# A one-core kernel of attention and two feed-forward layers: local attention regrouped from 64-key windows to blocks of 24 queries by 32 keys

## The chip, the core and the metric

The kernel runs on one core of one Trainium2 chip. The metric is the device time of one execution in microseconds (us). A core has TensorE (PE in the profile, its weight loads PEld), VectorE (DVE), ScalarE (ACT), GpSimd (POOL) and SyncE (SP, which here only issues DMAs). The engines run side by side and are kept in order by semaphores that the program counts by hand.

## What is computed

Attention of 4 batches x 8 heads, 576 positions, 64 wide, in two parts that are added; then two feed-forward layers over the 2304 tokens. Everything is fp32. Condensed:

```python
def _attn_ref(q, k, v):
    factor = 4; Sd = S // factor; scale = 1.0 / np.sqrt(D)
    q_d = q.reshape(B, H, Sd, factor, D).mean(axis=3)      # k_d, v_d alike
    out_d = sm_attn(q_d, k_d, v_d)                         # 144 x 144 softmax attention
    out_up = np.repeat(out_d, factor, axis=2)
    mask = np.abs(pos[:, None] - pos[None, :]) < factor    # local: 7 keys a query
    scores = np.where(mask, scale * q @ k.T, -1e9)
    out_local = softmax(scores) @ v
    return out_up + out_local
def _moe_ref(x, w_in, w_out):                              # 512 -> 2048 -> 512
    h = x @ w_in; return (h * tanh(softplus(h))) @ w_out   # Mish
def _moe2_ref(x, w_in, w_out, g_ln):                       # 512 -> 1024 -> 512
    h = x @ w_in; return (layernorm(h * softmax(h)) * g_ln) @ w_out
```

## The kernel before

**Stages.** Attention runs first, over 16 units (`UNITS`); a unit is two heads (2 x 64 = 128 partitions) of one batch. The first feed-forward layer follows in 6 tiles of 384 tokens by 16 blocks of hidden columns, then the second in 9 pairs of token tiles. Both layers are matmuls in fp32r, three per product (high and low parts), and their lines are not touched, save for the order of one Mish.

**Local attention of a unit.** A query sees the keys up to 3 positions away. The 576 queries are cut into 10 blocks of 58 (`QB`); each looks at a window of 64 keys (`KW`). `score_local` adds the mask into PSUM with 4 bf16 matmuls (L601), then computes 10 x 2 heads = 20 matmuls of 64 rows by 64 queries by 64 keys (L607) on the four 64x64 quarters of the array. In the profile an fp32 matmul that isn't a transpose has two records, so L607 shows 40 a unit. The scores of a unit are 128 x 640. VectorE takes the row maxima (L1099), subtracts them (L1102) and sums the exponentials (L1109); ScalarE exponentiates (L868); GpSimd normalises (L506). TensorE turns the result with 5 transposes (L631), ScalarE copies it (L863), and `value_local` multiplies by the values in `vw` with 20 matmuls of 64 keys by 64 columns by 58 queries (L657, 40 records). VectorE evicts in two copies of 128x290 (L1127).

**Pooled attention of a unit.** Queries, keys and values are summed in fours. GpSimd pools the queries (L485, L488), of every second unit also the keys; VectorE pools the other keys (L1064, 9 in all). GpSimd pools V from `v8`, 72 partitions of 8 rows each (L498, L499), so that each partition yields two pooled rows, g = 0 and 1. `score_pooled` is 6 matmuls (L588, 12 records), `turn_pooled` 6 transposes (L623), `value_pooled` 4 matmuls with 72 rows (L642, 8 records), two for each head.

**Order on TensorE.** It is written out by hand. In round u of 18 (`UNITS + LATE`) TensorE runs `turn_pooled` and `turn_local` of unit u-2, `score_local` and `score_pooled` of unit u, then `value_pooled` and `value_local` of unit u-2. In rounds 16 and 17, where there is nothing left to score, hidden blocks 0, 1 and 2 of the first layer (L671, 12 matmuls each) are put in.

**Order on the sync queue.** In round s: q and k of unit s (L405, L406), the values of unit s-3 into `vw` in 4 DMAs (L388) after a wait for `l_valued`, then `v8` of unit s-2 (L412) after a wait for `pool_v`.

**Mish.** ScalarE's `mish(0, 0)` stands in round 16; `mish(0, 1)` comes in the loop behind it, after weight block 4 and, because of `act.wait_ge(x_ok, UNITS)`, after the last eviction. There are two banks for hidden blocks, so `hidden(0, 3)` waits for `mish(0, 1)`.

Of the kernel before, what the change touches and what calls it, by code (L numbers as in the profile page):

```python
# [5 lines left out]
ALU = mybir.AluOpType  # L6
ACT = mybir.ActivationFunctionType
AX = mybir.AxisListType
# [17 lines left out]


KW = 64
QB = KW - 2 * (POOLF - 1)
NP = 5  # L30
NB = 2 * NP
PSTEP = 2 * QB - 1
LW = NP * KW

# [5 lines left out]
PQ = POOLED // 2  # L40
# [43 lines left out]
def first_query(i, jp):  # L84
    return PSTEP * i + QB * jp


def half_rows(h, jp):

    return slice((h ^ jp) * HD, (h ^ jp) * HD + HD)  # L90


def window(i, jp):

    return min(max(first_query(i, jp) - (POOLF - 1), 0), SEQ - KW)


def first_row(i, jp):

    return min(first_query(i, jp), SEQ - KW)  # L100

# [6 lines left out]
def program(nc, qT_d, kT_d, v_d, w1_d, w2_d, gln_d, out_d):  # L108
    with ExitStack() as ctx:
# [37 lines left out]
        v8 = sb("v8", [PQ, 2, 8 * P])  # L147
        qd = sb("qd", [P, 2, QPAD])
        kd = sb("kd", [P, 2, POOLED])
        vd = sb("vd", [PQ, 2, 2, P])  # L150
        half_qk = sb("half_qk", [P, 2, 2 * POOLED])
        half_v = sb("half_v", [PQ, 4 * P])
        band = sb("band", [P, 2, 2, KW], BF16)
# [4 lines left out]
        prob = sb("prob", [P, 2, NP, 2, KW])  # L158
        probT = sb("probT", [P, NP * P])
        pprob = sb("pprob", [P, 2, NPB, POOLED])  # L160
        vw = sb("vw", [P, 2, NP, P])
# [14 lines left out]
        pprobT = sb("pprobT", [PQ, 2, NPB, 2, PB])  # L176
        maskb = sb("maskb", [P, NB, KW], BF16)
        identb = sb("identb", [P, P], BF16)
        eps = sb("eps", [P, NB + NPB])
        mx = sb("mx", [P, 2, NP])  # L180

        den = sb("den", [P, 2, NB + NPB])
        rden = sb("rden", [P, 2, NB + NPB])
# [39 lines left out]

        SLB, SPB, PTB, OB = 0, 2, 3, 6
        TL0, TP1, OD0 = 512, 1024 + P, (NPB - 1) * PS + PR
# [7 lines left out]
        zero_ok = sem("zero_ok")  # L233
        ident_ok = sem("ident_ok")
# [8 lines left out]
        ld_v8 = [sem(f"ld_v8_{i}") for i in range(2)]  # L243
# [4 lines left out]
        pool_k = [sem(f"pool_k{i}") for i in range(2)]  # L248
# [19 lines left out]
        l_copied = sem("l_copied")  # L268
        l_valued = sem("l_valued")
        x_half = sem("x_half")  # L270
# [55 lines left out]
        VW_DMAS = 4  # L326
# [44 lines left out]
        def blocks(x):  # L371

            return x.rearrange("p b (i k) -> p b i k", i=NP)

# [5 lines left out]
        def _(sp):  # L380
            def load_windows(u):
                par = u % 2
                wait(sp, l_valued, u - 1)
                v_u = v_d[u]
                for jp, i0, n in ((0, 0, 1), (0, 1, NP - 1), (1, 0, NP - 1), (1, NP - 1, 1)):
                    src = bass.AP(v_u.tensor, v_u.offset + window(i0, jp) * P,
                                  [[P, KW], [PSTEP * P, n], [1, P]])
                    sp.dma_start(vw[jp * KW:(jp + 1) * KW, par, i0:i0 + n, :], src).then_inc(ld_vw[par], 16)  # L388
# [12 lines left out]
            for s in range(UNITS + 3):  # L401
# [5 lines left out]
                if s > 2:  # L407
                    load_windows(s - 3)
# [40 lines left out]
        def _(pool):  # L449
            n = [0]  # L450

            def own(ins):
# [10 lines left out]

            shift = POOLF - 1
            own(nc.gpsimd.memset(band[:], 0.0))
            own(nc.gpsimd.affine_select(out=band[:], in_=band[:], compare_op=ALU.is_ge, fill=MASKED,
                                        base=shift, pattern=[[-KW, 2], [shift, 2], [-1, KW]],
                                        channel_multiplier=1))
            nc.gpsimd.affine_select(out=band[:], in_=band[:], compare_op=ALU.is_ge, fill=MASKED,
                                    base=shift, pattern=[[KW, 2], [-shift, 2], [1, KW]],  # L470
# [4 lines left out]
            def pool_queries_keys(u):  # L475
# [4 lines left out]
                wait(pool, pool_k[0], (u + 1) // 2)  # L480
                halves = half_qk[:].rearrange("p a (i r) -> p a i r", r=2)
                both = ((qT, qd), (kT, kd))[:1 if u % 2 else 2]
                for a, (src, dst) in enumerate(both):
                    four = src[:, u % RQ, :].rearrange("p (i r) -> p i r", r=4)
                    ins = nc.gpsimd.tensor_tensor(halves[:, a], four[:, :, 0:2], four[:, :, 2:4], ALU.add)  # L485
                own(ins)
                for a, (src, dst) in enumerate(both):
                    nc.gpsimd.tensor_tensor(dst[:, par, 0:POOLED], halves[:, a, :, 0], halves[:, a, :, 1],  # L488
                                            ALU.add).then_inc((pool_q, pool_k[0])[a], 1)

            def pool_values(u):
                par = u % 2
                pool.wait_ge(ld_v8[par], 16 * (u // 2 + 1))
                wait(pool, p_valued, u - 1)
                wait(pool, pool_v, u)
                t2 = half_v[:, :].rearrange("p (g c) -> p g c", g=2)
                src = v8[:, par, :].rearrange("p (g c) -> p g c", g=2)
                own(nc.gpsimd.tensor_tensor(t2, src[:, :, 0:2 * P], src[:, :, 2 * P:4 * P], ALU.add))  # L498
                nc.gpsimd.tensor_tensor(vd[:, par, :, :], t2[:, :, 0:P], t2[:, :, P:2 * P], ALU.add)\  # L499
                  .then_inc(pool_v, 1)  # L500

            def normalise_local(u):
                par = u % 2
                pool.wait_ge(rden_ok, u + 1)
                rows = prob[:, par].rearrange("p i b k -> p (i b) k")
# [895 lines left out]
```

## Time and profile before

| | us |
|---|---|
| median of 3 runs | 713.41 |
| lowest, highest | 709.89, 714.75 |
| the profiled execution | 710.53 |
| its span | 708.7 |
| its mean granted clock | 0.995 |

| engine | busy us of the span | share |
|---|---|---|
| PE | 680.8 | 96% |
| PEld | 629.6 | 89% |
| DVE | 369.9 | 52% |
| ACT | 263.4 | 37% |
| POOL | 185.1 | 26% |

The page is read by stages. The first five or six of its 40 slices (17.7 us each) are attention; there DVE, ACT and POOL are busy eight to nine tenths, and DMA eight to nine. From the seventh slice on TensorE stands at nine tenths or more, and the others have slack. The change lies in the attention stage, so the shares of the whole span say little about it.

### The profile page before, as it was taken

What the parts mean: (1) busy time and instruction counts of PE and PEld (TensorE: products, weight loads), DVE (VectorE), ACT (ScalarE), POOL (GpSimd) and SP (SyncE); (2) the same over time, 40 slices, a digit from 0 to 9 for tenths busy, and PEclk for the clock granted to TensorE, in tenths of its full rate; (3) what the DMA queues carried; (4) which work ended last, traced back from release to release, by engine and by line L of the source; (5) the groups of instructions that cost most, each with busy time, mean ns of one, the idle gap of its engine ahead of it and who ended that gap; (6) DMA issues with size and microseconds to landing.
All of it is one profiled execution on the core that took longest, in us unless ns stands there. A gap on an engine that the chain in (4) does not pass through costs nothing.

```text
span 708.7 us, 12627 instructions
## 1 busy us (share of the span) xinstructions
PE 680.8 (96%) x5098; PEld 629.6 (89%) x5098; DVE 369.9 (52%) x686; ACT 263.4 (37%) x583; POOL 185.1 (26%) x228
## 2 busy tenths in 40 slices
PE   5879889999999999999999999999999999999998
PEld 4767679999999999999999999999778888888886
DVE  7999965642233223322232322564796667756671
ACT  5888764332112211221121122135564544444441
POOL 5999820000000000000000000584535434354100
PEclk9999999999999999999999999999999999999999
DMA  8999883000000000000000030002100000000001
GB/s 239 242 228 237 204 292 144 1 0 1 1 1 1 0 1 1 1 1 0 1 1 1 1 118 1 1 1 72 49 16 16 30 31 15 16 31 31 30 16 44
DMA packets 24185, 37.51 MB, mean 53 GB/s; under 512 B 2624, under 2 KB 12864, under 8 KB 24000
## 3 DMA queue, kind: packets, MB, share of 16 engines
q1 hardware_dynamic: 24128, 36.71, 17.8%
q8 instruction: 40, 0.66, 0.4%
q14 instruction: 17, 0.14, 0.1%
HBM read 31.99 MB, written 4.72 MB: 52 GB/s over the span
## 4 chain that ended last, share of the span: by engine, by line
PE 84%; POOL 7%; DVE 4%; issue 3%; DMA 1%; ACT 1%; SPq 0%; POOLq 0%; DVEq 0%; ACTq 0%
PE psum L671 28%; PE psum L685 28%; PE psum L777 12%; PE psum L754 11%; PE psum L763 2%; POOL half_v L498 2%; POOL half_qk L485 1%; POOL vd L499 1%; POOL prob L506 1%; POOL ylo L549 1%; DMA kT<-kT_dram 1%; POOL qd L488 1%; PE psum L657 1%; PE psum L642 1%; DVE so L1286 1%
## 5 line engine op out<-in xcount | busy, mean ns | idle before, releaser
L1183 DVE CAST ghi<-g_sb 128x384 fp32r<-128x384 f32 x96 | 39.7, 414 | 247.7 <-PE psum L685 190.8
L892 ACT ACTIVATE g_sb<-psum 128x384 f32<-128x384 f32 x96 | 47.2, 492 | 294.3 <-PE psum L671 290.6
L671 PE MATMUL psum<-xhi,whi 128*128 128x384 f32 x384 | 130.1, 339 | 2.5 <-ACT g_sb L892 2.2
L671 PE MATMUL psum<-xlo,whi 128*128 128x384 f32 x384 | 129.8, 338 | 0.0
L671 PE MATMUL psum<-xhi,wlo 128*128 128x384 f32 x384 | 129.7, 338 | 0.0
L685 PE MATMUL psum<-ghi,wlo 128*128 128x384 f32 x384 | 129.0, 336 | 0.0
L685 PE MATMUL psum<-ghi,whi 128*128 128x384 f32 x384 | 129.0, 336 | 0.0
L685 PE MATMUL psum<-glo,whi 128*128 128x384 f32 x384 | 129.0, 336 | 0.0
L521 POOL TENSOR_TENSOR t<-raw 128x1024 f32<-128x1024 f32 x1 | 2.6, 2640 | 352.9 <-PE psum L685 352.9
L671 PEld LDWEIGHTS psum<-xhi,whi 128*128 128x128 f32 x384 | 72.7, 189 | 3.0 <-ACT g_sb L892 2.3
L671 PEld LDWEIGHTS psum<-xhi,wlo 128*128 128x128 f32 x384 | 72.8, 190 | 0.0
L671 PEld LDWEIGHTS psum<-xlo,whi 128*128 128x128 f32 x384 | 72.6, 189 | 0.0
L685 PEld LDWEIGHTS psum<-ghi,whi 128*128 128x128 f32 x384 | 72.2, 188 | 0.1
L685 PEld LDWEIGHTS psum<-glo,whi 128*128 128x128 f32 x384 | 72.2, 188 | 0.1
L685 PEld LDWEIGHTS psum<-ghi,wlo 128*128 128x128 f32 x384 | 72.2, 188 | 0.0
L1187 DVE TENSOR_TENSOR glo<-g_sb,ghi 128x384 fp32r<-128x384 f32 x96 | 63.4, 660 | 3.3
L777 PE MATMUL psum<-whi,llo 128*128 128x512 f32 x144 | 57.2, 397 | 0.0
L777 PE MATMUL psum<-whi,lhi 128*128 128x512 f32 x144 | 56.7, 394 | 0.0
L777 PE MATMUL psum<-wlo,lhi 128*128 128x512 f32 x144 | 56.1, 390 | 0.0
L754 PE MATMUL psum<-whi,yhi 128*128 128x512 f32 x126 | 51.0, 405 | 2.3 <-POOL ylo L549 1.2
L754 PE MATMUL psum<-wlo,yhi 128*128 128x512 f32 x126 | 49.5, 393 | 0.0
L754 PE MATMUL psum<-whi,ylo 128*128 128x512 f32 x126 | 49.4, 392 | 0.0
(121 smaller groups left out, 1059.4 us busy)
## 6 DMA issues: line engine op xcount, KB each, us to landing
wraw<-w_dram SPq DMA_DIRECT2D x12, 512.0 KB, 7.8
qT<-qT_dram SPq DMA_DIRECT2D x16, 288.0 KB, 4.8
kT<-kT_dram SPq DMA_DIRECT2D x16, 288.0 KB, 7.4
v<-v_dram SPq DMA_DIRECT2D x16, 288.0 KB
out_dram<-ob SPq DMA_DIRECT2D x18, 256.0 KB, 2.0
vw<-v_dram SPq DMA_DIRECT2D x32, 128.0 KB, 4.7
wraw<-w_dram SPq DMA_DIRECT2D x16, 256.0 KB, 6.6
raw<-w_dram SPq DMA_DIRECT2D x1, 2048.0 KB, 7.4
```

What stands on the lines that cost most here:

```text
L485: ins = nc.gpsimd.tensor_tensor(halves[:, a], four[:, :, 0:2], four[:, :, 2:4], ALU.add)
L488: nc.gpsimd.tensor_tensor(dst[:, par, 0:POOLED], halves[:, a, :, 0], halves[:, a, :, 1], ALU.add).then_inc((pool_q, pool_k[0])[a], 1)
L498: own(nc.gpsimd.tensor_tensor(t2, src[:, :, 0:2 * P], src[:, :, 2 * P:4 * P], ALU.add))
L499: nc.gpsimd.tensor_tensor(vd[:, par, :, :], t2[:, :, 0:P], t2[:, :, P:2 * P], ALU.add)\
L671: ins = nc.tensor.matmul(bank, a[:, w], b[:, kdx, :], start=(kdx == 0 and n == 0), stop=(kdx == KD - 1 and n == 2))
L685: ins = nc.tensor.matmul(psum[:, YB + m, 0:N1], a[:, w], b[:, f % GR, :], start=(f == 0 and n == 0), stop=(f == F1 - 1 and n == 2))
L754: ins = nc.tensor.matmul(bank, a[p % 2][:, n, k, :], b[:, w], start=(k == 0 and m == 0), stop=(k == KH - 1 and m == 2))
L763: ins = nc.tensor.transpose(psum[:, T2B + c // 4, (c % 4) * P:(c % 4 + 1) * P], so[:, par, c * P:(c + 1) * P], ident[:])
L777: ins = nc.tensor.matmul(bank, a[:, par, c, :], b[:, w], start=(c == 0 and n == 0), stop=(c == F2 - 1 and n == 2))
L892: nc.scalar.activation(g_sb[:, f % HR, :], psum[:, HB1 + f % HB, 0:N1], ACT.Mish).then_inc(g_ok, 1)
L1183: nc.vector.tensor_copy(ghi[:, f % GR, :], g_sb[:, f % HR, :]).then_inc(ghi_ok, 1)
L1187: nc.vector.tensor_tensor(glo[:, f % GR, :], g_sb[:, f % HR, :], ghi[:, f % GR, :].bitcast(F32), ALU.subtract).then_inc(glo_ok, 1)
```

## The change

Local attention now works in 24 blocks (`NJ`) of 24 queries by 32 keys (`KW = 32`, `QB = 24`). The scores of a unit are 128 x 384 (12 groups of 32). Scoring is one mask matmul of 128x384 and 48 matmuls of 64 rows by 32 queries by 32 keys; score banks alternate between units. Turning takes 3 transposes. The values are multiplied by 48 matmuls of 32 keys by 64 columns by 24 queries, in two halves (keys in partitions 0 to 63, then 64 to 127), with `value_pooled` between the halves and a semaphore `l_half` ahead of the second. VectorE evicts a unit in one copy of 128x576. `vw` is loaded by 6 DMAs of 32 partitions instead of 4 of 64.

V for pooling lies as 4 rows to a partition over 128 + 16 partitions (`v4`, two DMAs), its unused part zeroed once; pooled attention is split into keys 0 to 127 and 128 to 143 (`PT = 16`) instead of two halves of 72. VectorE pools the keys of every unit. `mish(0, 1)` stands in round 17.

```diff
-KW = 64
-QB = KW - 2 * (POOLF - 1)
-NP = 5
+KW = 32
+QB = 24
+NJ = SEQ // QB
+NC = NJ // 4
+NA = NC // 2
+NG = 4 * NA
+LW = NG * KW
...
+def block_at(j):
+
+    return min(max(j * QB - (KW - QB) // 2, 0), SEQ - KW)
...
-        VW_DMAS = 4
+        VW_DMAS = 6
...
-                for jp, i0, n in ((0, 0, 1), (0, 1, NP - 1), (1, 0, NP - 1), (1, NP - 1, 1)):
+                for j, n in ((0, 1), (1, NC), (2, NC), (4, NC - 1), (3, NC - 1), (NJ - 1, 1)):
+                    r, c = j % 4, j // 4
+                    src = bass.AP(v_u.tensor, v_u.offset + block_at(j) * P, [[P, KW], [4 * QB * P, n], [1, P]])
+                    sp.dma_start(vw[r * KW:(r + 1) * KW, par, c:c + n, :], src).then_inc(ld_vw[par], 16)
...
-                    sp.dma_start(v8[:, u % 2, :], v_d[u].rearrange("(p t) c -> p (t c)", t=8))\
-                      .then_inc(ld_v8[u % 2], 16)
+                    sp.dma_start(v4[:, u % 2, 0, :], v_d[u][0:POOLF * P].rearrange("(p t) c -> p (t c)", t=POOLF))\
+                      .then_inc(ld_v4[u % 2], 16)
+                    sp.dma_start(v4[0:PT, u % 2, 1, :], v_d[u][POOLF * P:SEQ].rearrange("(p t) c -> p (t c)", t=POOLF))\
+                      .then_inc(ld_v4[u % 2], 16)
...
-                wait(pe, l_sub, u)
+                wait(pe, l_sub, u - 1)
+                nc.tensor.matmul(psum[:, SLB + par, 0:LW], identb[:],
+                                 maskb[:].unsqueeze(1).broadcast_to([P, NG, KW]), start=True, stop=False)
+                for j in range(NJ):
+                    r, jp, a = j % 4, j // 4 % 2, j // 8
+                    at, g = block_at(j), 4 * a + r
                     for h in range(2):
+                        rows, out = slice(h * HD, (h + 1) * HD), slice((2 * h + jp) * KW, (2 * h + jp + 1) * KW)
+                        ins = nc.tensor.matmul(psum[out, SLB + par, g * KW:(g + 1) * KW],
+                                               qT[rows, u % RQ, at:at + KW], kT[rows, u % RQ, at:at + KW],
+                                               start=False, stop=(a == NA - 1 and r == 3))
...
-                for g in range(2):
+                for g, n in enumerate((P, PT)):
                     for b in range(NPB):
+                        at = b * PS
+                        ins = nc.tensor.transpose(psum[0:n, PTB + 2 * g, at:at + PR], pprob[0:PR, par, b, g * P:g * P + n],
+                                                  ident[0:PR, 0:PR])
...
-                    for g in range(2):
-                        ins = nc.tensor.matmul(turned[rows, OD0:OD0 + POOLED], vd[:, par, g, rows],
-                                               pprobT[:, g, :, h, :], start=(g == 0), stop=(g == 1))
+                    for g, n in enumerate((P, PT)):
+                        ins = nc.tensor.matmul(psum[rows, PTB, OD0:OD0 + POOLED], vd[0:n, par, g, rows],
+                                               pprobT[0:n, g, :, h, :], start=(g == 0), stop=(g == 1))
...
+                for c in range(NC):
+                    for r in range(2 * half_, 2 * half_ + 2):
+                        keys, j = slice(r * KW, (r + 1) * KW), 4 * c + r
                         for h in range(2):
                             rows = slice(h * HD, (h + 1) * HD)
+                            q0 = c // 2 * P + (2 * h + c % 2) * KW + j * QB - block_at(j)
+                            ins = nc.tensor.matmul(psum[rows, OB + r % 2, j // 2 * QB:(j // 2 + 1) * QB],
+                                                   vw[keys, par, c, rows], probT[keys, q0:q0 + QB],
+                                                   start=True, stop=True)
+                ins.then_inc((l_half, l_valued)[half_], 1)
...
                 if u >= LATE:
+                    value_local(u - LATE, 0)
                     value_pooled(u - LATE)
-                    value_local(u - LATE)
+                    value_local(u - LATE, 1)
...
+                if u == UNITS + 1:
+                    mish(0, 1)
...
-                    if t > 0 or f > 0:
+                    if t > 0 or f > 1:
                         mish(t, f)
...
-                    if u % 2 == 0:
-                        pool_keys(u + 1)
+                    pool_keys(u + 1)
...
+            nc.vector.memset(psum[:, PTB + 2, 0:OD0], 0.0).then_inc(rest_ok, 1)
+            nc.vector.memset(v4[:, :, 1, :], 0.0).then_inc(rest_ok, 1)
```

## Rows read from the trace of the kernel before

**Rows 1.** Busy time of PE, PEld, DVE, ACT, POOL in 10 us; clock, DMA
```profile
40.00:50.00 10.00, 8.73 (x212) 7.25 (x216) 9.79 (x20) 8.58 (x26) 9.30 (x13) 1.00 1.00 233
```

**Rows 2.** Groups by line and shape, VectorE, 0 to 130 us: busy, mean ns
```profile
L1127 DVE COPY xy<-psum 128x290 f32<-128x290 f32 x32 | 13.7, 428 | 4.5 <-PE psum L657 4.2
...
L1102 DVE TENSOR_TENSOR prob<-psum,mx 128x640 f32<-128x640 f32 x16 | 13.2, 825 | 0.6
...
L1099 DVE TENSOR_REDUCE mx<-psum 128x10 f32<-128x640 f32 x16 | 12.9, 804 | 1.1 <-PE psum L607 1.1
...
L1090 DVE TENSOR_REDUCE psum<-psum 128x3 f32<-128x432 f32 x16 | 9.7, 605 | 0.0
...
L1064 DVE TENSOR_REDUCE kd<-kT 128x144 f32<-128x576 f32 x9 | 6.7, 741 | 0.0
```

**Rows 3.** The same view, GpSimd
```profile
L498 POOL TENSOR_TENSOR half_v<-v 72x512 f32<-72x512 f32 x16 | 22.0, 1374 | 0.5 <-DMA v<-v_dram 0.5
...
L506 POOL TENSOR_TENSOR prob<-prob,rden 128x640 f32<-128x640 f32 x16 | 20.1, 1259 | 8.4 <-DVE rden L1118 8.4
```

**Rows 4.** Chain that ended last, 46 to 53 us: start, us, what
```profile
46.54 0.73 PE psum L588 x11
47.27 0.65 PE psum L642 x8
47.92 0.74 PE psum L657 x40
48.66 0.73 PE psum L623 x6
49.39 0.55 PE psum L631 x5
49.94 0.26 PE psum L601 x4
50.20 0.58 PE psum L607 x39
50.78 2.00 issue
```

**Rows 5.** Groups by line and shape, TensorE, 0 to 130 us
```profile
L607 PE MATMUL psum<-kT,qT 64*64 64x64 f32 x640 | 13.9, 229 | 3.3 <-issue 3.2
```

**Rows 6.** Instructions in order of time, TensorE, 60 to 66 us: start, us
```profile
61.39 0.75 PE L607 MATMUL psum<-kT,qT 64*64 64x64 f32 x40
```

**Rows 7.** The same view, TensorE's weight loads; idle before them in brackets
```profile
61.23 0.11 PEld L601 LDWEIGHTS psum<-maskb,identb 64*64 64x64 bf16 x4 [0.17 <-issue]
63.28 0.45 PEld L642 LDWEIGHTS psum<-pprobT,vd 72*64 72x64 f32 x8 [0.20 <-issue]
```

**Rows 8.** DMA issues of the sync queue in order of time, 27 to 42 us
```profile
27.61 2.47 SPq L388 DMA_DIRECT2D vw<-v_dram  x4
...
31.61 0.33 SPq L405 DMA_DIRECT2D qT<-qT_dram  x1
31.98 0.43 SPq L406 DMA_DIRECT2D kT<-kT_dram  x1
...
41.43 0.55 SPq L412 DMA_DIRECT2D v<-v_dram  x1
```

**Rows 9.** Waits of the sync queue, 0 to 82 us: total, times, longest
```profile
SPq L412 <- POOL vd L499: 5.2, 7, 1.2
```

**Rows 10.** Waits of TensorE, 4 to 101 us
```profile
PE psum L607 <- issue: 3.2, 2, 2.0
```

**Rows 11.** TensorE in order of time, at the ends of the attention stage
```profile
11.58 0.80 PE L623 MATMUL psum<-ident,pprob 112*72 112x112 f32 x6 [0.42 <-ACT pprob L847]
...
99.81 0.81 PE L657 MATMUL psum<-probT,vw 64*64 64x58 f32 x40
...
102.81 0.50 PE L671 MATMUL psum<-xhi,whi 128*128 128x384 f32 x1 [2.19 <-ACT g_sb L892]
```

**Rows 12.** Stretch of 3.5 us after the last attention unit: busy, clock
```profile
103.00:106.50 3.50, 3.50 (x12) 3.50 (x12) 3.43 (x8) 2.20 (x5) 0.00 (x0) 0.51 1.03 403
```

More of the change, by code:

```diff
@@ L39 @@
 PS = 2 * HD
-PQ = POOLED // 2
+PT = POOLED - P
 QPAD = (NPB - 1) * PB + HD
@@ L242, in program @@
         ld_vw = [sem(f"ld_vw{i}") for i in range(2)]
-        ld_v8 = [sem(f"ld_v8_{i}") for i in range(2)]
+        ld_v4 = [sem(f"ld_v4_{i}") for i in range(2)]
         ld_wi = [sem(f"ld_wi{i}") for i in range(KD)]
@@ L247, in program @@
         pool_q = sem("pool_q")
-        pool_k = [sem(f"pool_k{i}") for i in range(2)]
+        pool_k = sem("pool_k")
         pool_v = sem("pool_v")
@@ L268, in program @@
         l_copied = sem("l_copied")
+        l_half = sem("l_half")
         l_valued = sem("l_valued")
-        x_half = sem("x_half")
         x_ok = sem("x_ok")
@@ L479, in pool_queries_keys @@
                 wait(pool, pool_q, u)
[L480 to L489, printed above, removed]
+                halves = half_q[:].rearrange("p (i r) -> p i r", r=2)
+                four = qT[:, u % RQ, :].rearrange("p (i r) -> p i r", r=4)
+                own(nc.gpsimd.tensor_tensor(halves, four[:, :, 0:2], four[:, :, 2:4], ALU.add))
+                nc.gpsimd.tensor_tensor(qd[:, par, 0:POOLED], halves[:, :, 0], halves[:, :, 1], ALU.add)\
+                  .then_inc(pool_q, 1)
             def pool_values(u):
                 par = u % 2
-                pool.wait_ge(ld_v8[par], 16 * (u // 2 + 1))
+                pool.wait_ge(ld_v4[par], 32 * (u // 2 + 1))
                 wait(pool, p_valued, u - 1)
                 wait(pool, pool_v, u)
[L496 to L499, printed above, removed]
+                src = v4[:, par]
+                own(nc.gpsimd.tensor_tensor(half_v[:], src[:, :, 0:2 * P], src[:, :, 2 * P:4 * P], ALU.add))
+                nc.gpsimd.tensor_tensor(vd[:, par, :, :], half_v[:, :, 0:P], half_v[:, :, P:2 * P], ALU.add)\
                   .then_inc(pool_v, 1)
@@ L640, in value_pooled, with value_local @@
                     rows = slice(h * HD, (h + 1) * HD)
-                    for g in range(2):
-                        ins = nc.tensor.matmul(turned[rows, OD0:OD0 + POOLED], vd[:, par, g, rows],
-                                               pprobT[:, g, :, h, :], start=(g == 0), stop=(g == 1))
+                    for g, n in enumerate((P, PT)):
+                        ins = nc.tensor.matmul(psum[rows, PTB, OD0:OD0 + POOLED], vd[0:n, par, g, rows],
+                                               pprobT[0:n, g, :, h, :], start=(g == 0), stop=(g == 1))
                 ins.then_inc(p_valued, 1)
-            def value_local(u):
+            def value_local(u, half_):
                 par = u % 2
-                pe.wait_ge(l_copied, u + 1)
-                pe.wait_ge(ld_vw[par], 16 * VW_DMAS * (u // 2 + 1))
-                wait(pe, x_ok, u)
-                for i in range(NP):
-                    for jp in range(2):
-                        keys = slice(jp * KW, (jp + 1) * KW)
+                if half_ == 0:
+                    pe.wait_ge(l_copied, u + 1)
+                    pe.wait_ge(ld_vw[par], 16 * VW_DMAS * (u // 2 + 1))
+                    wait(pe, x_ok, u)
+                else:
+                    pe.wait_ge(l_half, u + 1)
+                for c in range(NC):
+                    for r in range(2 * half_, 2 * half_ + 2):
+                        keys, j = slice(r * KW, (r + 1) * KW), 4 * c + r
                         for h in range(2):
                             rows = slice(h * HD, (h + 1) * HD)
-                            q0 = i * P + (h ^ jp) * HD + first_query(i, jp) - first_row(i, jp)
-                            ins = nc.tensor.matmul(psum[rows, OB + jp, i * QB:(i + 1) * QB], vw[keys, par, i, rows],
-                                                   probT[keys, q0:q0 + QB], start=True, stop=True)
-                ins.then_inc(l_valued, 1)
+                            q0 = c // 2 * P + (2 * h + c % 2) * KW + j * QB - block_at(j)
[3 more added lines that the diff above has]
+                ins.then_inc((l_half, l_valued)[half_], 1)
             def hidden(t, f):
@@ L862, in copy_local @@
                 wait(act, l_valued, u)
-                nc.scalar.copy(probT[:], turned[:, TL0:TL0 + NP * P]).then_inc(l_copied, 1)
+                nc.scalar.copy(probT[:], psum[:, PTB + 1, 0:LW]).then_inc(l_copied, 1)
             def exp_local(u):
@@ L1097, in subtract_local @@
                 dve.wait_ge(l_scored, u + 1)
-                scores = blocks(psum[:, SLB:SLB + 2, 0:LW])
+                scores = psum[:, SLB + par, 0:LW].rearrange("p (g k) -> p g k", g=NG)
                 nc.vector.tensor_reduce(mx[:], scores, AX.X, ALU.max).then_inc(l_max, 1)
```

142 lines of the change are left out of this document (51 added, 91 removed).

## The prediction

> **What bounds the kernel now.** I read the page first: attention fills its first hundred us, and behind it TensorE is busy nine tenths or more in work that the change leaves alone. So the question is how long attention takes. The table of stretches shows it [rows 1]: of 10 us VectorE is busy 9.79, GpSimd 9.30, PE 8.73, ScalarE 8.58, and the DMA engines all the time at 233 GB/s. VectorE, in its strict order, sets the pace. The turn of unit 0 starts at 11.58 [rows 11] and that of unit 7 at 48.66 [rows 4], so a unit takes 37.08 / 7 = 5.30 us. But TensorE is near: the chain of waits for one unit [rows 4] gives its blocks without a gap, 0.73 (L588) + 0.65 (L642) + 0.74 (L657) + 0.73 (L623) + 0.55 (L631) + 0.26 (L601) + 0.58 (L607) = 4.24 us, and then 2.00 us in which nothing in the profile holds it. The reader is to see four resources within a fifth of each other: whoever relieves one meets the next.
>
> **VectorE, what the change gives.** A reduce of 640 columns takes 804 ns and one of 432 columns 605 [rows 2], so a column costs 0.96 ns and 256 fewer save 0.25 us. Three instructions a unit shrink so (L1099, L1102 at 825 ns, L1109 like L1099): -0.74. Two copies of 428 ns become one with 286 columns more, 428 + 274 = 702: -0.15. Keys are pooled in every unit instead of every second one: 741 / 2 = +0.37. Together -0.52 us a unit, to some 4.8.
>
> **GpSimd, ScalarE.** Normalising goes from 640 to 384 columns, 1259 ns [rows 3] to about 0.76: -0.5; the keys leave it too. Pooling V keeps its 512 and 256 columns for a partition, only more partitions are used, so I leave L498 at 1374 ns; a gain there would be off the path. ScalarE's exponential and copy shrink likewise. None of the three is then at the front.
>
> **TensorE, what it costs.** Each block in turn.
> - L607 and L657 now have 48 matmuls instead of 20, 96 records instead of 40. What sets the price of one? The 40 of L607 stand in 0.75 us [rows 6], of which the last record's own 0.23 [rows 5] is tail: 0.53 over 9 steps, 0.059 us for a round of four, one on each quarter of the array. In L657 the moving side is 58 columns, not 64, and its 0.74 is still ten such rounds, 0.59, and 0.15 over. So the 64 stationary columns set the round, and the shorter moving side of 24 gains nothing.
> - L657: 24 rounds of 0.059 = 1.42 instead of 0.59: +0.83. With a round halved in spite of this, by its 24 columns, it would be +0.12; I take the first, since stationary stays at 64 columns.
> - L607: stationary and moving both fall to 32. Between a round halved (24 x 0.030 = 0.71) and a round unchanged (1.42) I take 0.95, near the lower end, because both sides are halved, a third up because eight matmuls in a row use the same two tiles. Against 0.58: +0.37, bounds +0.13 and +0.84.
> - L642: now its 8 records run two at a time, in 0.65 - 0.15 = 0.50. In the new form 128 rows and 16 rows alternate, and if different forms don't overlap they run one by one, 1.0: +0.49. Lower bound 0.
> - L631: three transposes instead of five of 0.11: -0.22. L623: three of its six load 128 columns instead of 72, +0.04. L601: one matmul on the whole array instead of four quarters at once, 0.
> - Changes of form. Where the tile form changes, weight loads stand idle 0.17 and 0.20 us [rows 7], and the block L657 has its 0.15 over. Between L623 and L631, of one form, there is none. Before, a unit has four such changes (into L623, L601, L642, L657). Now it has ten: into the 128-column turn, the 16-column turn, the local turn, the scores (64x32), the pooled scores (64x64), the first half (32x64), and four around the alternating 128 and 16 rows of `value_pooled`. Six more by 0.15: +0.90. If part of the wait overlaps, a third of it, +0.30; if all forms stay alike, 0.
>
> The Trainium skill, TensorEngine Tiling, section Key Properties, says that switching the tiling mode drains the engine; the trace agrees, with 0.15 over in L657. The same page, section Instruction Overhead, gives a matmul some 60 cycles whatever its length, and warns against taking a tiling factor from a dimension that is already small. By that a round of L607 would stay at 0.059, and the sum below would be 14 x 0.47 = 6.6 us higher; L657's 58 against L607's 64 columns at one pace speaks for it.
>
> Sum: 4.24 + 0.83 + 0.37 + 0.49 - 0.22 + 0.04 + 0.90 = 6.65 us a unit. Bounds: 4.24 + 0.12 + 0.13 - 0.22 + 0.04 + 0.30 = 4.6 at the low end, 4.24 + 0.83 + 0.84 + 0.49 - 0.22 + 0.04 + 1.20 = 7.4 at the high one. Only near the low end does TensorE stay under VectorE's 4.8. What waits behind it: every engine, since each round of TensorE carries both the scores of unit u and the values of unit u-2; the wait for `l_half` itself is covered by `value_pooled`. The evictions and copies that it waits for are shorter than before.
>
> **The sync queue.** Four `vw` issues take 2.47 us [rows 8], 0.62 each and 0.04 between. q and k take 0.33 and 0.43, `v` 0.55. Before: 2.64 + 0.85 + 0.59 = 4.1 a unit, and the queue had time to wait for `pool_v`, 5.2 us in 7 waits [rows 9]. After: 6 x 0.66 + 0.85 + 2 x 0.52 = 5.85, two `vw` issues and one `v` issue more. That is above the 5.30 of today, but under TensorE's 6.65, which hides it; if TensorE were cheaper, it would be the next bound. Smaller DMAs could issue faster: below, a unit's queue stays near 4.1 + 0.7 = 4.8 if the three added ones cost a third; above, 5.85 and the occasional long issue, 6.2. Bytes rise from 1.19 to 1.26 MB a unit; at 233 GB/s that is 5.4 us, also hidden at 6.65.
>
> **The stage.** From the turn of unit 0 at 11.58 to the end of the last L657 at 99.81 + 0.81 = 100.6 [rows 11] it takes 89.0 us. After: 14 rounds of 6.65 = 93.1; two rounds without scores, each 6.65 less L601 0.26, L607 0.95, L588 0.73 and its change 0.15, that is 4.56, together 9.1; three hidden blocks of 12 matmuls, 2.08 each by the chain, 6.2. The sum 108.4 puts the end at 120.0. TensorE also stops in the middle of L607 for nothing shown, twice, 3.2 us [rows 10]; with twice the instructions I add 2. The end comes at 122, or 21.4 later.
>
> **The start and Mish.** `hidden(0, 3)` waited 2.19 us for `mish(0, 1)` [rows 11], which now stands ahead of it: -2.2. In the 3.5 us after that idle time the granted clock was 0.51 (the lower of its two levels, 1.2 GHz) [rows 12]: without the gap those 3.5 us may run at 2.4 GHz, -1.7. VectorE's two zeroings at the start lie ahead of the masks, whose wait is for GpSimd; 0 to +1, taken as 0.
>
> Total: +21.4 - 2.2 - 1.7 = +17.5 on the profiled execution's 710.5 (its span 708.7 and 1.8 around it), 728.0. The median lies 2.9 above that execution, so 730.9, say 731.
>
> **Rivals.**
> - *VectorE stays the pace, faster.* If TensorE's unit costs under 4.8 us (changes of form at a third, short matmuls at half price in L657 too, `value_pooled` overlapped) and the sync queue under 4.8, the gain is VectorE's 0.52 x 16 = 8.3 and the 3.9 at the end: 713.4 - 12.2 = 701. For it: nobody can see in this trace what a 32-row tile costs. Against it: it needs four of my terms at their low ends at once, and cheaper DMA issues too.
> - *The sync queue sets the pace.* TensorE at 5.8 or less, the queue at 5.85: 0.55 x 16 = 8.8 more, less 3.9: 718. For it: the issue rows are steady. Against it: two of TensorE's terms must be near their low ends.
> - *The change doesn't do what it says.* TensorE and queue both near 5.3, VectorE's gain unused: 713 less 3.9, 710.
> - *Worse.* All upper bounds, 7.4 a unit: 16 x 0.75 = 12 more and further stops in L607: 743 to 752. The stops of 2.00 us could double in number.
>
> **How the numbers follow.** TensorE as summed: 0.66, own range 721 to 742. The queue at 718 or nothing moving: 0.13. Faster: 0.12. Worse than 742: 0.09. Within 1% is 706 to 720.5, about what a measurement can tell from no change. So faster 0.12, same 0.13, slower 0.75. The range 708 to 745 leaves the faster case and the upper part of the worst one out.
>
> **What would show it.** PE's chain for a unit should sum to 6 to 7 us, with L657's successor twice 0.7; weight loads with 10 idle stretches of 0.15 a unit; VectorE busy some 7 of 10 us with waits for PE; the sync queue with few waits. If instead VectorE is still above 9 of 10, the changes of form or the short matmuls are cheaper than I took them, and the prediction is wrong by the first rival. If PE waits for DMAs into `vw`, it is the second.

## The result, and the profile after

| | before | after |
|---|---|---|
| median of 4 runs, us | 712.47 | 746.21 |
| lowest, highest | 709.89, 714.75 | 740.77, 747.24 |
| profiled execution, its span | 710.53, 708.7 | 745.98, 744.2 |
| first pooled turn to last matmul of `value_local` | 11.58 to 100.40 = 88.8 | 11.99 to 137.83 = 125.8 |
| of it at the lower clock (1.2 GHz) | 3.4 | 37.5 |
| from the next hidden matmul to the end of the span | 605.9 | 605.9 |

The changed kernel is slower: 1.0447 of before, interval 1.0407 to 1.0487. All of it lies in the attention stage, 37.0 us longer; the wait behind it is 2.0 us shorter, and what follows is the same to a tenth. The prediction had the sign and the engine right (TensorE becomes the bound). 731 was 15 us too low, and the time lies 1.2 us above its range.

First the stretch that answers to [rows 1], in the table of stretches of the changed kernel (busy us and instructions of PE, PEld, DVE, ACT, POOL in 10 us; granted clock as a share of 2.4 GHz; DMA share; GB/s):

```profile
40.00:50.00 10.00, 10.00 (x213) 7.61 (x206) 3.99 (x10) 3.73 (x13) 3.94 (x6) 0.50 0.50 147
50.00:60.00 10.00, 8.89 (x316) 6.97 (x313) 5.81 (x12) 3.74 (x14) 4.02 (x5) 0.99 0.53 154
60.00:70.00 10.00, 10.00 (x334) 8.12 (x333) 6.34 (x15) 6.52 (x24) 3.91 (x6) 0.83 0.57 180
```

VectorE falls from 9.79 to between 4 and 6.3, GpSimd from 9.30 to 4, DMA from 233 GB/s to 150 to 180: whatever shared the bound before now waits. PE is the only full engine, and from 40 to 50 it is full at half speed: 10.00 busy, clock 0.50. That column is what I had not counted on.

The chain of waits answers to [rows 4]. The first ten rows are at the lower clock, the rest at the higher one (lines of the changed kernel: L600 `turn_pooled`, L608 `turn_local`, L580 mask, L587 scores, L571 `score_pooled`, L638 `value_local`, L619 `value_pooled`):

```profile
40.65 2.25 PE psum L619 x7
42.90 0.23 PE psum L638 x11
43.13 0.09 PE psum L619
43.22 0.87 PE psum L638 x35
44.09 1.31 PE psum L600 x6
45.41 0.64 PE psum L608 x3
46.05 0.32 PE psum L580
46.36 1.80 PE psum L587 x96
48.17 1.63 PE psum L571 x12
49.80 0.99 PE psum L638 x48
...
52.85 0.72 PE psum L600 x6
53.57 0.33 PE psum L608 x3
53.90 0.16 PE psum L580
54.07 1.19 PE psum L587 x77
55.25 0.88 PE psum L571 x12
56.13 0.74 PE psum L638 x41
56.88 1.11 issue
57.99 0.31 PE psum L638 x7
58.30 1.33 PE psum L619 x7
59.63 0.14 PE psum L638 x11
59.76 0.04 PE psum L619
59.80 0.56 PE psum L638 x35
```

Without its stop ("issue", in which TensorE stands still and the profile shows nothing that it waits for) a unit takes 0.72 + 0.33 + 0.16 + 1.19 + 0.88 + 0.82 + 1.33 + 0.14 + 0.04 + 0.56 = 6.17 us at the higher clock (0.82 is the first half of `value_local` where no stop parts it, as at 88.13 us; here it stands as 0.74 and 0.31). At the lower clock, from the turn at 44.09, it is 1.31 + 0.64 + 0.32 + 1.80 + 1.63 + 0.99 + 2.25 + 0.23 + 0.09 + 0.87 = 10.1 us, the last four taken from the rows ahead of that turn. The turns and the mask grow by 1.8 to 2.0 times, the scores by 1.5. So each us at the lower clock makes a unit 0.39 us longer: the one from 44.02 to 52.78, with 6.1 us of it and no stop, took 8.76, and 6.17 + 6.1 x (1 - 6.17 / 10.1) is 8.5.

The waits of TensorE, 4 to 139 us (total, times, longest), answer to [rows 10]:

```profile
PE psum L587 <- issue: 4.6, 4, 2.2
PE psum L580 <- DMA kT<-kT_dram: 4.3, 1, 4.3
PE psum L638 <- issue: 3.1, 4, 1.3
```

Within the stage TensorE waits for no other engine: the 4.3 us for its first keys and two waits for ScalarE (0.4 and 0.6) lie ahead of it, and one of 0.2 behind. What stands there is "issue", nothing that a semaphore shows: 7.7 us.

The groups by line and shape of the changed kernel, 0 to 140 us (busy us, mean ns), answer to [rows 2, 3, 5]:

```profile
L638 PE MATMUL psum<-probT,vw 32*64 32x24 f32 x1536 | 33.4, 223 | 3.1 <-issue 3.1
...
L587 PE MATMUL psum<-kT,qT 64*32 64x32 f32 x1536 | 24.8, 213 | 4.6 <-issue 4.6
...
L481 POOL TENSOR_TENSOR half_v<-v 128x512 f32<-128x512 f32 x16 | 21.0, 1313 | 0.0
...
L1106 DVE COPY xy<-psum 128x576 f32<-128x576 f32 x16 | 11.2, 703 | 7.1 <-PE psum L638 7.1
...
L1086 DVE TENSOR_TENSOR prob<-psum,mx 128x384 f32<-128x384 f32 x16 | 8.9, 557 | 0.6
L1083 DVE TENSOR_REDUCE mx<-psum 128x12 f32<-128x384 f32 x16 | 8.8, 553 | 16.8 <-PE psum L587 16.7
```

The 703 ns of the eviction is the 702 of the prediction, and the VectorE instructions at 553 and 557 (the third, the sum, takes 552) are each a quarter us shorter, as worked out. VectorE's gain is there in full; it is spent waiting for the scores.

### The profile page after: what moved, and what is told of

Same layout as the page of the kernel before. It is cut to its first block, busy times and chain, and to the rows that moved or that the text cites. A ratio compares the mean times of both kernels' runs of the same rounds, so it can differ in the third digit from the quotient of the medians.

```text
span 744.2 us, 16055 instructions
## 1 busy us (share of the span) xinstructions
PE 724.4 (97%) x6810; PEld 660.9 (89%) x6810; DVE 357.6 (48%) x679; ACT 253.9 (34%) x583; POOL 170.2 (23%) x214
## 4 chain that ended last, share of the span: by engine, by line
PE 94%; DVE 2%; issue 2%; POOL 1%; ACT 1%; DMA 0%; SPq 0%; DVEq 0%
PE psum L653 27%; PE psum L667 27%; PE psum L761 12%; PE psum L738 11%; PE psum L638 4%; PE psum L619 3%; PE psum L587 3%; PE psum L571 2%; PE psum L600 2%; PE psum L747 2%; PE psum L608 1%; POOL ylo L532 1%; DVE so L1263 1%; PE psum L580 0%; DMA kT<-kT_dram 0%
```

## The experiments

Two questions were open: which blocks of TensorE were mis-sized, and where the lower clock and the stops come from. For each kernel below the stage is measured as in the table above, from one profiled execution each. Four executions of the changed kernel alone lie 6.5 us apart, with mean granted clocks of 0.972 to 0.988, so differences of 2 us between two stages say little by themselves; the time of a block and the place of a stop can be read from one trace.

| kernel | ratio to before, interval | stage | of it at 1.2 GHz |
|---|---|---|---|
| a_vp | 1.0387 (1.0326 to 1.0449) | 119.2 | 34.1 |
| a_sc | 1.0458 (1.0394 to 1.0521) | 123.6 | 37.5 |
| a_vpsc | 1.0406 (1.0370 to 1.0443) | 120.4 | 41.0 |
| a_v8 | 1.0424 (1.0355 to 1.0492) | 125.7 | 34.1 |
| a_fill8 | 1.0500 (1.0438 to 1.0562) | 127.9 | 23.9 |
| a_nomish | 1.0505 (1.0455 to 1.0555) | 125.9 | 37.5 |
| b_mish | 0.9970 (0.9947 to 0.9993) | 91.3 | 6.8 |
| b_keys | 1.0005 (0.9978 to 1.0032) | | |
| b_mk | 1.0012 (0.9993 to 1.0031) | 90.8 | 3.4 |
| b_v4 | 1.0004 (0.9979 to 1.0029) | 90.6 | 0.0 |
| b_dup | 1.0588 (1.0561 to 1.0616) | 128.3 | 37.5 |
| b_big | 1.0102 (1.0068 to 1.0135) | 95.2 | 0.0 |

Kernels in a_ are the changed kernel with one edit (a_vpsc with two), those in b_ the kernel before with one (b_mk with two).

### The order in value_pooled (a_vp)

```diff
-                for h in range(2):
-                    rows = slice(h * HD, (h + 1) * HD)
-                    for g, n in enumerate((P, PT)):
+                for g, n in enumerate((P, PT)):
+                    for h in range(2):
+                        rows = slice(h * HD, (h + 1) * HD)
```

> The changed kernel with the two loops of value_pooled swapped: both heads' matmuls over the 128 rows first, then both over the 16 rows. Theory A (a unit costs what TensorE's blocks add up to): two of the four changes of tile form go, 0.15 us each, and the heads' matmuls run two at a time again, 8 records in 0.5 instead of 1.0 us, so 0.6 to 0.8 us a unit and 10 to 12 us in all, about 735. Rival B (the stretches at the lower clock are the cost): they stay, and the gain is small, under 4 us. Rival C (the sync queue or VectorE sets the pace): no change.

Measured: 739.80 us, and the stage 6.6 us shorter. The chain of waits of this kernel:

```profile
55.92 0.57 PE psum L619 x5
56.49 0.14 PE psum L638 x11
56.63 0.04 PE psum L619
```

`value_pooled` takes 0.57 (and 0.04) instead of 1.33: the two heads' matmuls on 128 rows run at once, then the two on 16 rows, with one change of form instead of three. So the alternation was worth 0.76 us a unit, about the 0.79 (0.49 and two changes at 0.15) that the prediction gave it. Sixteen times 0.76 would be 12.2; the stage gave back only 6.6, because the stops "issue" went from 7.7 to 13.5 us.

### The order of the scores, and both orders (a_sc, a_vpsc)

```diff
-                for j in range(NJ):
-                    r, jp, a = j % 4, j // 4 % 2, j // 8
-                    at, g = block_at(j), 4 * a + r
+                for n in range(NJ):
+                    a, r, jp = n // 8, n // 2 % 4, n % 2
+                    j, g = 8 * a + 4 * jp + r, 4 * a + r
+                    at = block_at(j)
```

> The changed kernel with the 48 score matmuls in another order, so that four in a row go to four different tiles instead of two. Theory A, with the round priced by tiles in use: L587 falls from 1.19 to about 0.9 us at the full clock, 0.3 us a unit, about 741. If TensorE already overlaps all four tiles in the old order, or if a matmul has a floor however short, no change (within 1 us). Rival C: no change.

Measured: 744.49. The 48 matmuls of the scores take 0.85 to 0.95 us instead of 1.19 at the higher clock and 1.44 instead of 1.80 at the lower: four in a row on four tiles is cheaper than eight on two. The stage is 2.2 us shorter, where 16 x 0.24 to 16 x 0.34 is 3.8 to 5.4. Both orders together:

> The changed kernel with both orders of its TensorE work mended: value_pooled goes through both heads over the 128 rows and then both over the 16, and the scores go so that four in a row use four tiles. Nothing is left out. Apart, they took 6.6 and 2.2 us off the stage. If the unit's blocks alone count, 8 to 10 us less than the changed kernel, 737 us. If what TensorE saves in blocks comes back as stops, as with the old V split, 739 to 743 us. In either case not below 735: the orders are a part of the loss only.

Measured: 739.74, no less than a_vp alone, with 14.8 us of stops and 41.0 us at the lower clock. The second saving does not show in the time; there are 1.3 us more of stops than in a_vp and 6.9 us more at the lower clock. That was the hint to look at them and not at the blocks.

### The V split alone, both ways (a_v8, b_v4)

a_v8 is the changed kernel with the old `v8` and two halves of 72 keys; b_v4 is the kernel before with `v4` and the split 128 + 16. Its core:

```diff
-                    for g in range(2):
-                        ins = nc.tensor.matmul(turned[rows, OD0:OD0 + POOLED], vd[:, par, g, rows],
-                                               pprobT[:, g, :, h, :], start=(g == 0), stop=(g == 1))
+                    for g, n in enumerate((P, PT)):
+                        ins = nc.tensor.matmul(turned[rows, OD0:OD0 + POOLED], vd[0:n, par, g, rows],
+                                               pprobT[0:n, g, :, h, :], start=(g == 0), stop=(g == 1))
```

> The changed kernel with one part undone: V for pooling on 72 partitions, two halves of 72 keys, one DMA, no zeroing. Theory A: value_pooled costs 0.65 again instead of 1.33 us, three changes of form less there and two less at the 16-column turn: 0.9 to 1.2 us a unit, 14 to 19 us, about 730. Rival B: the clock still falls, gain under 5 us. Rival C, if the sync queue is the bound: one issue less, 0.47 us a unit, 7 us.

Measured: 743.31. The blocks get shorter as in a_vp, but the stage does not. The chain of waits of a_v8 (L585 scores, L636 `value_local`):

```profile
50.41 0.40 PE psum L585 x18
50.80 2.03 issue
52.84 1.00 PE psum L585 x61
...
55.46 2.69 issue
```

Two stops in one unit, 4.7 us together, in the midst of matmuls that wait for nobody. The expectation was wrong here: `value_pooled` takes 0.65 us instead of 1.37, 16 x 0.72 = 11.5 us, and the stops grow from 7.7 to 17.3 us; the stage is no shorter.

> The kernel before with only the pooled attention split into 128 and 16 keys and V for pooling on 128 + 16 partitions. Theory A: value_pooled rises by 0.7 us and six changes of form become ten or so: TensorE's unit goes from 4.2 to about 5.2, just at VectorE's 5.3, so the kernel gets 0 to 10 us slower, 718 taken. If VectorE alone sets the pace: no change, below 1 us. GpSimd's pooling of V at 1374 ns stays within 5%.

Measured: 713.54. Here `value_pooled` takes 1.55 to 1.59 us, TensorE's unit grows from 4.24 to 5.29 by the distance of two turns (45.04 and 50.33), and TensorE is full. The two rows of its chain around `value_pooled`, and one stretch of 10 us:

```profile
47.89 0.12 issue
48.01 1.59 PE psum L648 x8
```

```profile
50.00:60.00 10.00, 9.92 (x214) 7.42 (x206) 9.30 (x19) 8.05 (x25) 9.38 (x12) 1.00 0.87 240
```

PE 9.92 of 10, clock 1.00, no stop over 0.12 in these units. A full TensorE alone brings neither the lower clock nor the stops.

### Large matmuls as filling (a_fill8)

```diff
+                for _ in range(8):
+                    nc.tensor.matmul(psum[:, SLB + par, LW:512], identb[:], identb[:], start=True, stop=True)
```

The eight bf16 matmuls stand ahead of the mask in each unit; nobody reads them and the output is the same.

> The changed kernel with 8 matmuls of 128x128x128 bf16 added ahead of each unit's mask matmul, into unused columns of the score bank; nobody reads them, the output is unchanged. They cost about 8 x 0.056 = 0.45 us a unit at the full clock, 7 us in all. Theory A alone: 7 us slower, 753. Rival B: if what TensorE does in attention is what lets the clock fall, full-array matmuls keep it up in part, the 37 us at 0.50 shrink and the total stays at 746 or falls to as low as 738.

Measured: 747.58, stage 127.9, of it 23.9 at the lower clock. 16 x 0.45 = 7.2 us of work were added and the stage grew by 2.1, while 13.6 us less ran at the lower clock; at 6.17 against 10.1 us a unit these are 13.6 x (1 - 6.17 / 10.1) = 5.3 us. One trace against one is weak here: the changed kernel's own execution of 740.77 us had a mean clock of 0.988 too. Over all four executions the mean clock is 0.986 with the filling and 0.977 without, so it seems to help the clock, and the time is no better.

### Many small or few large matmuls (b_dup, b_big)

Both add work to TensorE in the kernel before, with no 32-row form and no new change of form; nobody reads it and the output is the same.

```diff
+                for _ in range(14):
+                    for jp in range(2):
+                        for h in range(2):
+                            nc.tensor.matmul(psum[half_rows(h, jp), SLB + jp, LW:LW + 24],
+                                             qT[h * HD:(h + 1) * HD, u % RQ, 0:KW],
+                                             kT[h * HD:(h + 1) * HD, u % RQ, 0:24], start=True, stop=True)
```

> The kernel before, with 56 more matmuls a unit (64 stationary rows and columns, 24 moving columns, on the four quarters of the array in turn, like its own scores) ahead of the mask; their result is read by nobody, the output is the same. The count of matmuls a unit is then about that of the changed kernel, but all of them keep the 64x64 form and no change of form is added. 28 rounds of 0.059 are 1.65 us: TensorE's unit goes to about 5.9. If the lower clock and the stops of the changed kernel come from how many small matmuls a unit has, this kernel shows them too: 20 us or more at half clock within the stage, stops well above the 3.2 us of before, and 732 to 740 us. If they hang on the 32-row forms or on the changes of form, the clock stays at 1.00 as in the variant with the V split alone, the stage grows by 16 x 0.7 = 11 us, and the time is 722 to 726 us.

```diff
+                for _ in range(5):
+                    nc.tensor.matmul(psum[:, SLB, LW:512], ident[:], qT[:, u % RQ, 0:192], start=True, stop=True)
```

> The kernel before with five large matmuls a unit ahead of the mask (128 stationary columns, 192 moving columns, on the whole array), 10 records instead of the 112 of the variant with small ones, and about as much time: I estimate 1.5 to 2.3 us a unit, to a TensorE unit of 5.8 to 6.5. Their result is read by nobody, the output is the same. If the clock falls and the stops appear because TensorE is so long without idle time, this kernel shows 20 us or more at half clock and several stops, and 735 to 750 us. If they hang on the number of small matmuls, the clock stays at 1.00 in nearly all of the stage and no stop over 0.5 us appears, and the time is 713 + 16 x (0.5 to 1.2) = 721 to 732 us.

Measured: b_dup 752.23, b_big 718.26. One stretch each, b_dup first, b_big behind it:

```profile
50.00:60.00 10.00, 9.06 (x192) 8.16 (x193) 2.96 (x8) 2.68 (x9) 4.26 (x5) 0.52 0.30 89
```

```profile
50.00:60.00 10.00, 10.00 (x203) 8.89 (x201) 9.70 (x19) 7.86 (x26) 7.22 (x8) 1.00 0.73 214
```

The waits of TensorE in b_dup, 4 to 130 us (L600 are the added matmuls):

```profile
PE psum L613 <- issue: 4.7, 3, 2.9
...
PE psum L600 <- issue: 3.3, 3, 1.5
PE psum L588 <- issue: 2.9, 2, 2.1
PE psum L663 <- issue: 2.8, 3, 2.1
```

b_dup shows all that the changed kernel shows: 37.5 us at the lower clock, 14.5 us of stops, an even longer stage. b_big has none of it: TensorE is busy 10.00 of 10 in every stretch from 20 to 90 us, the clock stays at 1.00 and no stop "issue" is listed. b_big's unit stands in its chain as 1.63 + 0.26 + 0.58 + 0.73 + 0.65 + 0.74 + 0.73 + 0.55 = 5.87 us. In b_dup's chain at the higher clock the added block and the mask behind it are

```profile
101.34 1.76 PE psum L600 x112
103.10 0.14 PE psum L607 x4
```

and the unit is 1.76 + 0.14 + 0.58 + 0.73 + 0.65 + 0.74 + 0.73 + 0.55 = 5.88 us. So the two kernels give TensorE the same work in time, to 0.01 us a unit, and one has a stage of 95.2 us and the other of 128.3. It is not the 32-row form, not the changes of form, and not how full TensorE is. It is how many small matmuls it runs. The 28 added rounds took 1.76 / 28 = 0.063 us each, near the 0.059 expected.

### What TensorE waits for in the stops

The trace also records the DMA packets that bring instructions. In the page's part on the queues (packets, MB, share of 16 engines) they stand, for the changed kernel, as

```profile
q8 instruction: 54, 0.88, 0.5%
```

against 40 packets and 0.66 MB before: 0.88 MB / 54 = 16 KB each. Within the stage they come every 5.85 us before, every 4.67 after, 4.73 in b_dup, 5.86 in b_big. They are TensorE's: all its records (matmuls, weight loads and semaphore waits) divided by the packets of the whole execution give 260 before, 256 after, 259 in b_dup and 255 in b_big. Read from the single packet records of that queue, the six stops of the changed kernel over 0.4 us and five of b_dup stand like this:

```
kernel   stop begins  length  last q8 packet began  work resumes, us
         us           us      before the stop, us   after that packet's end
after    22.9         1.32    0.99                  0.98
after    36.7         1.64    1.07                  1.37
after    56.9         1.11    1.53                  1.36
after    70.2         0.48    1.72                  1.25
after    78.7         0.46    2.01                  1.41
after    100.9        2.20    0.34                  1.44
b_dup    18.3         2.92    -0.59                 1.36
b_dup    48.8         2.11    0.49                  1.43
b_dup    72.2         2.13    0.90                  1.60
b_dup    88.0         1.49    0.77                  1.34
b_dup    103.6        1.41    1.01                  1.55
```

However long the stop, work resumes 1.0 to 1.6 us after the end of a packet of instructions. The seven a_ kernels (the changed one among them) and b_dup have 74 stops of more than 0.4 us in their stages. Two of them, at 15.2 us in a_vpsc and at 15.5 in a_nomish, the profile puts down to a `vw` DMA; the other 72 are "issue", and all of them end 0.98 to 1.66 us behind such a packet. Their place is stricter still. Count all of TensorE's records in the trace from the start of the kernel and divide by 256: 71 of the 72 stops stand where the remainder is 193, and the last where it is 195. So they stand at the border of a block of 256 instructions, whatever matmul is at work there. In the kernel before three stops do, those at 44.9, 50.8 and 80.8 us, and these are the three longest entries "issue" among its waits, the 2.00 of [rows 4] with them. Its other gaps are waits for GpSimd and VectorE, and four of at most 0.9 us ahead of the pooled scores, put down to "issue" too, which stand at other places (remainders of 25 and 113 for the two longest) and whose cause I don't know. b_v4 and b_big have no such stop. So TensorE has run out of instructions: it has reached the end of a block and the next one has not come.

What makes them late is how fast they are used up. The records a unit, weight loads counted too: 230 before (115 and as many loads), 444 after, 454 in b_dup, 250 in b_big; by the units' lengths that is 43, 72, 77 and 43 a us. At 43 the packets come in time. Before, where other waits part the units, TensorE runs at 230 / 4.24 = 54 a us in between, and three packets were late. At 72 and 77 many are. At the lower clock the changed kernel uses 444 / 10.1 = 44 a us, and only 3 of the 72 stops begin there, though 28% of the stages' time is at that clock. Crowded DMA engines are not the cause: their busy share from 50 to 60 us is 0.30 in b_dup and 0.73 in b_big. In a_v8, with a still shorter unit, the packets are later still, and this is why the gains in the blocks came back as stops. The Trainium skill, Runtime: NRT & Kernel Launch, section Instruction fetch mechanics, says that an engine's instructions are fetched in blocks of 16 KiB, 256 instructions, ahead of use and mostly hidden. The size and the count agree with the packets here; that the fetch is hidden holds at 43 a us and not at 72.

**And the clock.** Many stretches at the lower clock begin shortly after such a stop starts: in the changed kernel five of the six within the stage, 2.1 to 3.9 us behind it, in b_dup all four, 1.4 to 2.1 us behind, in before the one at 82.6, 1.7 us behind. Over the seven a_ kernels and b_dup it is 31 of 42 within 4 us, and the longer stops are followed more often: 14 of 17 over 1.6 us, 4 of 19 under 0.8. But three of the 42 (a_sc at 18.0 us, a_nomish at 18.9 and 29.1) have no such stop ahead of them at all, and the stops of 2.00 us in before at 50.8 and of 1.49 in b_dup at 88.0 were followed by none. That the idle time of the stops pulls the clock down is thus likely in part, and argued only: no kernel here had the stops without the many small matmuls, which may act on the clock by themselves. The cause of the lower clock stays open. The Trainium skill, TensorE: Matmul & The Clock Gate, section HAM oscillation, ties the lower clock to idle time of TensorE; here it stayed on through ten us in which PE was busy 10.00 of 10.

### Mish and the keys (a_nomish, b_mish, b_keys, b_mk)

a_nomish takes `mish(0, 1)` back to its old place; b_mish makes this edit in before, b_keys lets VectorE pool the keys of every unit in before, b_mk does both.

```diff
+                if u == UNITS + 1:
+                    mish(0, 1)
...
-                    if t > 0 or f > 0:
+                    if t > 0 or f > 1:
```

```diff
-                both = ((qT, qd), (kT, kd))[:1 if u % 2 else 2]
+                both = ((qT, qd),)
...
-                    if u % 2 == 0:
-                        pool_keys(u + 1)
+                    pool_keys(u + 1)
```

> The changed kernel with the second Mish back where it was. The gap before hidden(0, 3) was 2.19 us before and 0.8 now: 1 to 3 us slower than the changed kernel, 748.

Measured: 748.46 to the 746.21 of the changed kernel, the intervals overlapping. In the profiles the matter is plain; TensorE in order of time, first the changed kernel, then a_nomish:

```profile
138.29 0.45 PE L653 MATMUL psum<-xhi,whi 128*128 128x384 f32 x1 [0.25 <-ACT g_sb L875]
```

```profile
140.19 0.69 PE L653 MATMUL psum<-xhi,whi 128*128 128x384 f32 x1 [1.89 <-ACT g_sb L875]
```

The wait of 1.89 us is down to 0.25. The stretch at the lower clock behind it stays: from 138.9 to 142.3 us in the changed kernel, from 138.4 to 145.2 in a_nomish.

> The kernel before with only the second Mish put ahead, into round 17. If hidden(0, 3) starts 2.2 us earlier and the 3.5 us at half clock behind the gap go too: 3.9 us faster, 708.6. If only the gap goes: 2.2. If what is next (the weight blocks of output(0, 0)) takes the gap over: within 1 us of before. In the changed kernel 0.6 us of waiting was left at this place.

Measured: 710.34 against 712.68, ratio 0.9970 (0.9947 to 0.9993). But in its profile the first hidden matmul behind the stage starts at 103.02, before at 102.81: the gap is closed because attention ends later, the last `value_local` at 102.75 and not 100.40. That trace has a stop of 3.03 us at a block border at 50.5 us, and the stage is 2.5 us longer. So the profile does not show the 2 us.

> The kernel before with the keys of every unit pooled by VectorE. If VectorE sets the pace of the kernel before: 0.37 us more a unit over 16, less the POOL work that goes, 5 to 6 us slower, 718. If GpSimd sets it (the chain runs over it at 55 to 79 us): faster by up to 0.5 x 16 = 8 us. If TensorE: no change.

Measured: 712.85, against 712.68. The profiled execution of this kernel took 3814 us, so its trace is not used. 16 x 0.37 = 5.9 us more on VectorE cost nothing: VectorE was not the strict pace of before.

> The kernel before with the second Mish ahead and the keys of every unit pooled by VectorE; nothing is left out. GpSimd loses some 0.8 us a unit, VectorE gains 0.37. If VectorE paced the kernel before, 713 - 2 + 5 = 716 us. If the pace was shared, so that the two shift nothing, as the keys alone measured: 710 to 711 us, the same as with Mish alone.

Measured: 710.97 against 710.89, so the gain of b_mish did not show again beside the keys. Whether Mish ahead is worth 2 us or nothing in the kernel before stays open; it is at most 0.5%.

## Why the prediction was right in its sign and short in its size

**VectorE and GpSimd.** The gains were as worked out, save normalising (835 ns, not 760) and V pooling (1313, not 1374). But "VectorE sets the pace" at 5.30 was too strong: the keys alone should then have cost 5.9 us and cost nothing, and b_v4 ran at the same 5.29 with TensorE full. The forecast of 731 does not hang on it, since it puts TensorE at 6.65; the first two rivals do.

**TensorE's blocks.** The sum 6.65 was 0.48 too high.

| term | predicted us | measured us |
|---|---|---|
| L657, now L638 in two halves | 1.57 | 0.82 + 0.14 + 0.56 = 1.52 |
| L607, now L587 | 0.95 | 1.19 |
| L642, now L619 | 1.14 | 1.33 + 0.04 |
| L631, now L608 | 0.33 | 0.33 |
| L623, now L600 | 0.77 | 0.72 |
| L601, now L580 | 0.26 | 0.16 |
| L588, now L571 | 0.73 | 0.88, with its change of form |
| six more changes of form | 0.90 | in the rows above |

The short moving side indeed gained nothing in `value_local`. The scores stood above my 0.95 because of the order on the tiles: 0.85 to 0.95 with it mended. The changes of form were the term that was too large. Only the one into `score_pooled` (0.15) and those in `value_pooled` show; without its 0.90 the sum was 5.75, so that changes and errors of the blocks together make 0.42.

**The sync queue.** Six `vw` issues took 2.71 to 4.13 us, where 6 x 0.66 was 3.96: one takes 0.44 in the median, with some of over a us among them, against 0.62 before. The queue was never near: it waited 25.1 us in 12 waits for `value_local`. The rival that it sets the pace fell by this.

**The stage, the step that failed.** Predicted 110.4 us from the first turn (108.4 and 2 for stops), measured 125.8. With the measured blocks the same sum is 14 x 6.17 + 2 x (6.17 - 0.16 - 1.19 - 0.88) + 6.2 = 100.5, which is 7.9 under the forecast's 108.4. Against that stand 37.5 x (1 - 6.17 / 10.1) = 14.6 us for the lower clock, which had no term at all, and 7.7 for stops, where I had 2. The sum is 122.8. The other 3.0 of the 125.8 lie in the units that have a stop or lower clock, 0.1 to 0.5 us in each; the unit from 117.57 us, which has neither, took 6.17. The prediction said "with twice the instructions I add 2" and looked for the stops in L607 alone. It saw the right rows, [rows 10] and the 2.00 of [rows 4], and did not ask what they were: the same stops as after, from instructions that came too late, seen three times in the kernel before. It also took 1.00 in [rows 1] for granted, though the same view of the kernel before shows a fall within the stage:

```profile
80.00:90.00 10.00, 8.60 (x170) 7.61 (x171) 9.10 (x16) 6.68 (x19) 7.07 (x8) 0.83 0.54 139
```

**Mish and the start.** The gap of 2.2 us went, as predicted. The -1.7 for a better clock behind it did not come. Together: 15.4 too little for the stage, 1.7 for the clock behind it, 0.4 for the later start and some 0.4 for what is left of the gap: 17.9 of the 18.0 between 728.0 and 745.98.

**The page on tiling.** The prediction weighed the rule of the Trainium skill, TensorEngine Tiling, section Instruction Overhead, by which a round of L607 would stay at 0.059 and the block take 1.42. The trace lies between: 1.19 / 24 = 0.050 a round as written, 0.035 to 0.040 with four tiles in turn.

## What to carry to other kernels

Cutting a matmul into smaller ones costs more than the sum of their times: TensorE must also be fed, and here 43 instructions a us came in time while 72 often did not. Count the instructions of a unit, weight loads too, divide by its length, and when the chain shows "issue" in the midst of matmuls that wait for nobody, compare it with the packets of instructions before working on any block. And read the clock column in every stretch: a unit of 6.17 us became one of 10.1 there.

## What the runs showed of the hardware that I had not expected

- TensorE stopped for up to 2.9 us in the midst of a row of small matmuls, and went on 1.0 to 1.7 us after the end of a 16 KB packet of instructions; all 72 stops stand at the border of a block of 256 instructions. The same work in time as large matmuls (b_big) ran without a stop.
- The clock stood at 1.2 GHz through ten us with PE busy 10.00 of 10 (40 to 50 us), in a kernel with stops of 0.5 to 2.2 us; with eight large matmuls a unit added it was there 13.6 us less in the profiled execution.
- Matmuls of 128 and 16 rows in turn, for one head after the other, took 1.33 us; first both heads on 128 rows and then both on 16 took 0.57.
- An issue of a `vw` DMA took 0.44 us for 32 partitions, 0.62 for 64 (medians).
- Pooling V by GpSimd over 128 partitions took 1313 ns, over 72 partitions 1374, with the same 512 columns.
